# The down projection of two mixtures of experts: three 192-column matmuls that add into one PSUM region, in place of one of 384 and one of 192

## What is computed

```
x = conv(x)                                  # 14336 tokens, 192 values each
# layer 0: only tokens with x @ w_skip > 0; layer 1: all tokens
e    = argmax(x @ w_gate)                    # layer 1 adds a bias by modality
h    = relu(x @ w1[e])                       # 192 -> 1024, "up"
y    = gate * (h @ w2[e])                    # 1024 -> 192, "down"
out  = x + y   (layer 0)      out = y   (layer 1)
```

## Time and profile before

| | |
|---|---|
| Times of three runs | 1259.74, 1263.01, 1268.81 us (median 1263.01) |
| Span of the profiled execution | 1261.0 us |
| PE busy | 1154.4 us (92%), 8677 matmul records |
| PEld busy | 1134.5 us (90%) |
| DVE / ACT / POOL busy | 625.7 (50%) / 489.1 (39%) / 465.4 us (37%) |
| Mean granted TensorE clock | 0.911 of full speed |

### The profile page before, as it was taken

How to read it: one execution, slowest core, us unless ns; L and a number is a source line. 1 busy time by engine, 2 the same in 40 slices (tenths; PEclk the granted TensorE clock), 3 DMA queues, 4 the chain that set the end, 5 groups by cost and what they waited for, 6 DMA issues and landing times. The chain is left out here.

```text
span 1261.0 us, 27560 instructions
## 1 busy us (share of the span) xinstructions
PE 1154.4 (92%) x8677; PEld 1134.5 (90%) x8678; DVE 625.7 (50%) x1896; ACT 489.1 (39%) x879; POOL 465.4 (37%) x576
## 2 busy tenths in 40 slices
PE   1999998289999999999982999999999999999997
PEld 1998998289999999999982999999999999999997
DVE  1356647426666666666662544444444444444444
ACT  0555545124343444444431433333333333333333
POOL 3177567612332323423331432233332332322334
PEclk7667757559999999999995999999999999999999
DMA  5244434444414334244124311111111111111110
GB/s 122 68 118 136 123 103 117 129 117 106 143 41 135 87 110 119 79 117 118 46 57 132 97 39 45 39 42 42 39 39 45 39 42 42 39 44 40 39 45 27
DMA packets 85561, 97.91 MB, mean 78 GB/s; under 512 B 26719, under 2 KB 76211, under 8 KB 85535
## 3 DMA queue, kind: packets, MB, share of 16 engines
q1 hardware_dynamic: 68362, 67.04, 20.6%
q0 software_dynamic: 15072, 28.47, 6.7%
q10 hardware_dynamic: 2100, 2.09, 0.5%
HBM read 65.79 MB, written 33.54 MB: 79 GB/s over the span
## 5 line engine op out<-in xcount | busy, mean ns | idle before, releaser
L915 PE MATMUL p_h<-xt,w_up 128*128 128x256 f32 x3600 | 461.0, 285 | 13.2 <-ACT xt L987 6.9
L915 PEld LDWEIGHTS p_h<-xt,w_up 128*128 128x128 f32 x3600 | 448.3, 190 | 18.4 <-ACT xt L987 9.2
L928 PE MATMUL p_y<-w_dn,hid_hi 128*128 128x384 f32 (+1 forms) x1440 | 447.2, 371 | 0.2 <-DVE hid_lo L1106 0.2
L1008 ACT ACTIVATE hid_hi<-p_h 128x512 fp32r<-128x512 f32 x360 | 215.0, 598 | 514.5 <-PE p_h L915 512.1
L924 PE MATMUL p_y<-w_dn,hid_lo 128*128 128x192 f32 (+1 forms) x1440 | 352.4, 255 | 0.0
L1106 DVE SCALAR_TENSOR_TENSOR hid_lo<-p_h,hid_hi 128x512 fp32r<-128x512 f32 x360 | 247.1, 690 | 209.2 <-ACT hid_hi L1008 208.7
L924 PEld LDWEIGHTS p_y<-w_dn,hid_lo 128*128 128x128 f32 x1440 | 275.8, 192 | 0.0
L928 PEld LDWEIGHTS p_y<-w_dn,hid_hi 128*128 128x128 f32 x1440 | 272.4, 189 | 1.2 <-DVE hid_lo L1106 0.4
L862 POOL DMA_INDIRECT out<-y_out,idx x114 | 112.3, 985 | 243.9 <-DVE y_out L1099 223.4
L855 POOL TENSOR_TENSOR split<-ahead,split 128x256 fp32r<-128x256 f32 x94 | 64.3, 684 | 300.8 <-ACT split L991 300.7
L455 POOL DMA_INDIRECT buckets<-rows,idx x128 | 125.7, 982 | 68.8 <-issue 50.3
(11 more groups left out here) (193 smaller groups left out, 1297.7 us busy)
## 6 DMA issues: line engine op xcount, KB each, us to landing
ahead<-buckets SPq DMA_DIRECT2D x94, 202.0 KB, 2.4
x_in<-in_x SPq DMA_DIRECT2D x16, 672.0 KB
stage<-in_w SPq DMA_DIRECT2D x11, 768.0 KB
kept<-buckets SPq DMA_DIRECT2D x33, 202.0 KB, 2.6
stage<-in_w SPq DMA_DIRECT2D x11, 512.0 KB
stage<-in_w SPq DMA_DIRECT2D x22, 256.0 KB
x_in<-in_w_t SPq DMA_DIRECT2D x9, 512.0 KB, 7.2
x_in<-in_w_t SPq DMA_DIRECT2D x9, 256.0 KB, 8.0
```

Of the source, the lines that this page charges most:

```text
L915: mm = nc.tensor.matmul(o, w_up[:, slot, w, f * P:(f + 1) * P], xt[:, a * UNIT:(a + 1) * UNIT], start=(m == 0), stop=(m == len(terms) - 1))
L928: mm = nc.tensor.matmul(p_y[:, t, 0:2 * COLS], hid_hi[:, f, c], w_dn[:, slot, f, :, 0:COLS], start=(f == 0), stop=(f == FT - 1))
L1008: nc.scalar.activation(hid_hi[:, 2 * b:2 * b + 2, :], p_h[:, b % HB, :].rearrange("p (f c) -> p f c", f=2), ACT.Relu).then_inc(hi_done, 1)
```

## The change

`down` now issues three matmuls of `COLS` columns for each f and t: `hid_hi` x high, `hid_hi` x low, `hid_lo` x high, all into `p_y[:, t, 0:COLS]`. The second half of the region is not written. The first of the 24 matmuls of a group starts the sum, the last one ends it. `finish` is left with one DVE instruction for each t, straight from `p_y` to `y_out` or `rows1`; the buffer `y_lo` and the semaphore steps between the two DVE passes are gone.

```diff
 def down(f, slot):
     for t in range(SUBS):
-        c = slice(t * P, (t + 1) * P)
-        def lo_times_hi():
-            nc.tensor.matmul(p_y[:, t, 0:COLS], hid_lo[:, f, c], w_dn[:, slot, f, 0, 0:COLS], start=False, stop=False)
-        if f == FT - 1:
-            lo_times_hi()
-        mm = nc.tensor.matmul(p_y[:, t, 0:2 * COLS], hid_hi[:, f, c], w_dn[:, slot, f, :, 0:COLS], start=(f == 0), stop=(f == FT - 1))
-        if f < FT - 1:
-            lo_times_hi()
+        c, o = slice(t * P, (t + 1) * P), p_y[:, t, 0:COLS]
+        terms = ((hid_hi, 0), (hid_hi, 1), (hid_lo, 0))
+        for m, (hid, w) in enumerate(terms):
+            mm = nc.tensor.matmul(o, hid[:, f, c], w_dn[:, slot, f, w, 0:COLS], start=(f == 0 and m == 0),
+                                  stop=(f == FT - 1 and m == len(terms) - 1))
         if f == FT - 1:
             mm.then_inc(y_ready, 1)
@@ finish
     for t in range(SUBS):
         dve.wait_ge(y_ready, g * SUBS + (t + 1))
         if last:
-            ins = nc.vector.tensor_scalar(y_lo[:, t, 0:D], p_y[:, t, D:2 * D], gate[t], None, ALU.mult)
+            ins = nc.vector.tensor_scalar(y_out[:, t, :], p_y[:, t, 0:D], gate[t], None, ALU.mult)
         else:
-            ins = nc.vector.scalar_tensor_tensor(y_lo[:, t, :], p_y[:, t, COLS:2 * COLS], gate[t], kept[:, t, 0:COLS], ALU.mult, ALU.add)
-        ins.then_inc(dve_chain, 1)
-    for t in range(SUBS):
-        dve.wait_ge(dve_chain, t + 1)
-        to = y_out[:, t, :] if last else rows1[:, t, 0:COLS]
-        ins = nc.vector.scalar_tensor_tensor(to, p_y[:, t, 0:COLS], gate[t], y_lo[:, t, 0:COLS], ALU.mult, ALU.add)
+            ins = nc.vector.scalar_tensor_tensor(rows1[:, t, 0:COLS], p_y[:, t, 0:COLS], gate[t], kept[:, t, 0:COLS], ALU.mult, ALU.add)
     ins.then_inc(y_read, 1)
-    dve.sem_clear(dve_chain)
```

More of the change, by code:

```diff
@@ L162, in conv_two_moes @@
         dest_f = sb("dest_f", [P, SUBS])
-        y_lo = sb("y_lo", [P, SUBS, D + E])
         y_out = sb("y_out", [P, SUBS, D])
```

## The result

The changed kernel takes 1317.8 us (median; 1315.8 to 1322.8), the kernel before 1263.0. The ratio is 1.0445 with a 95% interval of 1.0403 to 1.0486: slower by 54.8 us. The forecast was 1313 us, with 1300 to 1352 as range. The profiled execution has a span of 1317.9 us, 56.9 above that of before.

What follows compares the result with a forecast made beforehand. TensorE was taken as the bound, its down matmuls becoming load-bound. Terms 37.0 + 16.5 + 0.6 - 3.5 - 0.75 gave +49.9 us: 1310.9 from the profiled 1261.0, 1313 us as median; range 1300 to 1352.

Steps and rivals of the forecast that it cites:

- The mechanism: Down matmuls: three loads per f and t, 0.110 us each, cannot hide: 0.330 us against 0.288 for the old pair.
- rival 1: Down matmuls: streaming decides and loads are always hidden, three matmuls take 0.279 us, total 1248 us; chance 0.04.
- rival 2: Down matmuls: the second `hid_hi` matmul needs no new load, 0.279 us a triple, total 1248 us; chance 0.05.
- rival 3: Down matmuls: load and stream overlap less well, each step costs 0.120 us like up matmuls, total 1352 us; chance 0.12.
- Layer 1, forecast +37.0: Layer 1 down stretches grow from 4.67 to 5.33 us, +0.66 in 56 units, the last one's extra being hidden.
- Layer 0, forecast +16.5: Layer 0 down stretches grow from 4.93 to 5.43 us, +0.50 in each of 33 units.
- The lower clock, forecast +0.6: Part of layer 0's first down stretch, at 1.2 GHz: +0.10 instead of +0.04 us for about ten pairs.
- Rival 4: Down stretches: the clock falls to 1.2 GHz, a triple takes 0.64 us, far over 1400 us if all units; chance 0.03.
- The waits, forecast -3.5: Layer 0: longer down stretches fill seven PE waits for ACT's `xt`, 0.5 us given back at each.
- DVE, forecast -0.75 at one place: Hand-over at layer 0's end: two of four `finish` instructions go, saving 0.75 us; in the units this is hidden.

Runs made afterwards that it cites:

- e3: Changed kernel, but layer 1's down matmuls except the first of a group move only 96 columns: 1411.5 us (one run), kernel before 1299.2 on that chip.
- e4: Changed kernel in another order, with nearly all layer 1 down matmuls moving 256 columns, not 192: 1370.0 us (one run), kernel before 1299.2 in that chip's runs.
- e10: Kernel before with its 384- and 192-column down matmuls grouped four and four over two slices: 1263.6 us, ratio 1.0012 to the kernel before.
- e11: Kernel before with grouped down matmuls, `hid_lo` and its moving weights in bfloat16: 1248.1 us against 1263.6, ratio 0.9845.
- e1: Changed kernel with `hid_lo` x high placed between the two `hid_hi` matmuls: 1358.8 us against 1299.2 for the kernel before on that chip, ratio 1.0466.
- e2: Changed kernel, but the low product goes into the second half of `p_y` and DVE reads twice as before: 1363.5 us, kernel before 1299.2, ratio 1.0474.
- e6: Kernel before with the three-matmul change in layer 1 only: 1343.2 us, ratio 1.0305 to the kernel before, +40.9 us.
- e7: Kernel before with the three-matmul change in layer 0 only: 1318.7 us, ratio 1.0117 to the kernel before, +16.4 us.
- e9: Kernel before with only DVE's part changed, one read of `p_y`, low product left out; repeat run: 1260.8 us against 1263.6, ratio 0.9965.

## Why the prediction was right, point by point

**The mechanism.** For the down matmuls it held: each of the three loads its 128 columns, loads are evenly spaced, 48 of them fill a stretch, and the second `hid_hi` has one of its own. e3 shows the same step with half the columns, e4 a slightly longer one at 256, e10 that the order is no matter, e11 that the operand type is. Rivals 1, 2 and 3 fall by the row of 0.112 us, by the "x2" of `hid_hi` and e1, and by the step being 0.112 and not 0.120; e2 takes away the reason given for rival 3. One reading went too far: that 0.11 us is the least distance of two loads of 128 columns. The transposes just ahead of the earlier trace rows have such loads too, and there six steps take 0.52 us, under 0.09 each. Timeline of PEld, before:

```profile
990.72 0.14 PEld L904 LDWEIGHTS p_xt<-ident_r,split 128*128 128x128 f32 x1
...
991.24 0.19 PEld L928 LDWEIGHTS p_y<-w_dn,hid_hi 128*128 128x128 f32 x1
```

So 0.112 us is the step of the down products' loads, not of every load of 128 columns. What the rows show is the spacing; a matmul's record starts before its load's ends.

**Layer 1, forecast +37.0, measured +42.5 less 0.7 at the end.** The size of one term was off: I took 0.110 us a step, between 0.109 and 0.112, and the chain runs at 0.112. The 0.109 was the distance of a single pair of loads behind a long matmul; the two readings of a chain, 0.112 from the logits' loads scaled to 128 columns and 0.112 from the one extra matmul, were right. That makes 0.08 us in each of 56 units, 4.5 us. The remaining 1 us is outside the down stretches: on average over the 56 units a unit grew by 0.76 us and its down stretch by 0.74.

**Layer 0, forecast +16.5, measured +0.64 in a later unit, 20.5 over 32 units.** 0.08 of the 0.14 missed is the step again. The other 0.06 is a slip in the sum: I charged all 24 wider columns of a pair, though by the prediction's own mechanism the 8 of the short matmul cost nothing. Only 16 x 16 columns / 2.4 GHz = 0.107 us are the wider matmuls, which leaves 0.155 and not 0.10 for `r_ranks`, and 5.57 - 5.41 = 0.16 is what it takes after.

**The lower clock, forecast +0.6 in the first unit.** The first down stretch took its small extra (14.24 instead of 13.21 us, +1.0 where 0.5 + 0.6 were forecast), but two other first units of segments ran partly at 1.2 GHz, +6.3 us, which no term held. Rival 4 thus happened in small. Whether the change makes it likelier is open: half-clock stretches inside layer 0, beyond one that is under way at its start, add up to 3.4 to 17.1 us in the six profiles with the new down products there, and to 0 to 13.7 us in the seven with 384-column ones. The means are 10 and 5 us, but the ranges overlap, and e6 and e7 have the same 3.4.

**The waits, forecast -3.5, measured -5.0 for `xt`.** They went from 6.9 to 1.9 us: the stretch grew by 0.64 and not by 0.50, which is 4.5 us over seven waits, and they scatter (1.6 to 4.4 us in the profiles with the new layer 0). Three new waits with no releaser shown ("issue", 1.8 us) stand elsewhere, at the start of segments.

**DVE, forecast -0.75 at one place, measured at three.** At the hand-over 40.04 + 0.64 - 39.78 = 0.9 us were saved; the hand-overs of the five profiles with three matmuls and one pass of DVE in layer 0 run from 39.6 to 40.2, so it is 0.5 to 1.1. Two steps failed here. One is the end: I said that POOL's weight split, which hides the last down stretch, leaves the end alone. It does hide the stretch; but POOL reaches that split by way of the scatter of the unit before, which waits for DVE, so 0.65 us were saved there. The other is layer 0: I said that DVE's saving is hidden in the units because PE's next wait on `y_read` lies 40 up matmuls later. PE also waits for `hid_lo`, which DVE makes behind `finish`, from the 31st up matmul on. In the seven units behind a segment's first the up parts fell from 40.8 to 37.3 us in the changed kernel too, where the table of waits before had 1.5 us for `hid_lo` in all. Longer waits for `xt` can take part of that back, as in e9.

**The sum.** 49.9 us were forecast; the stretches above give 42.5 + 20.8 - 0.3 - 0.7 = 62.3 us, less 5.4 us ahead of layer 0 that the change did not make. Layer 0's 20.8 is 20.5 of longer stretches, 6.3 of clock, -5.0 and +1.8 of waits and some -3 of shorter up parts. The median moved by 54.8, and e6 and e7 add up to 57.3. With 0.112 us a step the prediction's own sum was about +58. That this comes so near is in part luck: it holds neither the clock nor DVE's -3 us nor the +1.8.

## What to carry to other kernels

Before a wide matmul is cut into narrow ones with the same stationary operand, count the loads: here each float32r matmul of 96 to 200 moving columns with a load of 128 columns took 0.112 us, one of 256 took 0.119, and one of 384 about 0.18 (a pair's 0.288 less 0.112), so narrow ones did not cost less for streaming less. Fewer reads on an engine that mostly waits gave back 3 to 5 us of 1263, at the few places where that engine was late; they show when the same unit is compared from start to start in both traces, not in its share of busy time. Where narrow matmuls cannot be avoided and precision allows, give them an operand type with a short load and put them next to each other (e11).

## What the runs showed of the hardware that was not expected

Loads in a chain: 0.112 us at 2.4 GHz for 128 float32r columns whether 96 or 192 columns stream behind each; 0.119 for 256; in the transposes under 0.09. Four matmuls of 192 columns take 0.29 us together with bfloat16 operands (995.17 to 995.46 in e11) and 0.42 with float32r ones (997.27 to 997.69 in e10). The Trainium skill (TensorE: Matmul & The Clock Gate, LDWEIGHTS) gives columns / 1.2 as a load's nanoseconds, an estimated 0.107 us for 128; a chain of float32r loads shows 0.112. The Trainium skill (same page, Weight-path perf modes) has a faster load for operands that are not FP32; e11's rows agree, with records of 98 ns against 190.

TensorE's clock can fall while its records show no gap: in e3 it was at 1.2 GHz for half of the time from 785 to 880 us with PE and PEld busy all through, when the down matmuls moved 96 columns, and at 2.4 GHz throughout the same layer with 192. So taking streaming out of a TensorE-bound stage made it some 50 us longer.
